# The last attention step's transposed probabilities in a bank and a buffer of their own, and one PSUM copy moved from ScalarE to VectorE

## Time and profile before

| | |
|---|---|
| median of 3 runs | 1077.67 us (1076.57 to 1077.71) |
| profiled execution, its own time | 1077.91 us |
| its span, first to last instruction | 1076.3 us |
| PE busy | 1057.4 us, 98% of the span |
| DVE busy | 344.9 us, 32% |
| ACT busy | 356.3 us, 33% |
| POOL busy | 393.1 us, 37% |

### The profile page before, as it was taken

One profiled execution on the slowest core, in us unless ns is written; L12 is line 12 of the kernel. 1 busy time (PEld: TensorE's weight loads), 2 busy tenths in 40 slices (PEclk: granted clock), 3 DMA queues, 4 the chain that ended last, 5 costly groups with the idle time before them and its releaser, 6 DMA issues.

```text
span 1076.3 us, 17647 instructions
## 1 busy us (share of the span) xinstructions
PE 1057.4 (98%) x5848; PEld 884.3 (82%) x5849; DVE 344.9 (32%) x700; ACT 356.3 (33%) x821; POOL 393.1 (37%) x310
## 2 busy tenths in 40 slices
PE   8999979999999999999999999999999999999998
PEld 6888758888888888888888887988888888888886
DVE  5878841112211122111221112332333232333222
ACT  4678432222222222222222221533344334335333
POOL 6223178785827346280462806830010001100000
PEclk9999999999999999999999999999999999999999
DMA  6676645949733325133241412240011002101001
GB/s 190 175 258 183 219 139 195 331 145 351 245 117 117 117 83 170 39 117 117 79 174 39 149 67 69 88 128 20 20 51 48 20 1 79 40 1 40 1 1 40
DMA packets 50195, 120.09 MB, mean 112 GB/s; under 512 B 7072, under 2 KB 12320, under 8 KB 49632
## 3 DMA queue, kind: packets, MB, share of 16 engines
q0 software_dynamic: 16688, 62.66, 17.8%
q1 hardware_dynamic: 19920, 32.62, 9.7%
q10 hardware_dynamic: 13536, 24.12, 6.5%
HBM read 86.88 MB, written 32.51 MB: 111 GB/s over the span
## 4 chain that ended last, share of the span: by engine, by line
PE 92%; DVE 3%; ACT 2%; DMA 1%; issue 1%; ACTq 0%; POOL 0%; SPq 0%; DVEq 0%; POOLq 0%
PE bank L1492 7%; PE bank L1494 7%; PE bank L1511 7%; PE bank L1509 7%; PE bank L1493 7%; PE bank L1510 7%; PE bank L1557 6%; PE bank L1559 6%; PE bank L1558 6%; PE bank L1550 6%; PE bank L1552 6%; PE bank L1551 6%; PE bank L1517 3%; PE bank L1284 2%; PE bank L1476 2%; PE bank L1310 2%
## 5 line engine op out<-in xcount | busy, mean ns | idle before, releaser
L482 POOL TENSOR_TENSOR Wl<-stage,Wh 128x2048 fp32r<-128x2048 f32 x36 | 165.8, 4605 | 3.0
L1161 DVE COPY y_out<-bank 128x512 f32<-128x512 f32 x42 | 29.1, 692 | 355.2 <-PE bank L1511 355.2
L1492 PE MATMUL bank<-Wh,xT_h 128*128 x336 | 135.4, 403 | 1.4 <-issue 0.9
L1199 DVE SCALAR_TENSOR_TENSOR bank<-bank,square 128x512 f32<-128x512 f32 x72 | 50.4, 700 | 254.8 <-ACT square L837 254.8
L1494 PE MATMUL bank<-Wh,xT_l 128*128 x336 | 131.5, 391 | 0.0
L1511 PE MATMUL bank<-Wh,hT_l 128*128 x336 | 131.1, 390 | 0.0
L1509 PE MATMUL bank<-Wh,hT_h 128*128 x336 | 130.9, 390 | 0.1
L1510 PE MATMUL bank<-Wl,hT_h 128*128 x336 | 130.8, 389 | 0.0
L1493 PE MATMUL bank<-Wl,xT_h 128*128 x336 | 130.8, 389 | 0.0
L808 ACT ACTIVATE hT_h<-bank 128x512 fp32r<-128x512 f32 x84 | 45.8, 596 | 252.3 <-PE bank L1517 252.3
L480 POOL CAST Wh<-stage 128x2048 fp32r<-128x2048 f32 x36 | 68.5, 1903 | 157.2 <-PE bank L1511 155.1
(11 more groups left out here) (236 smaller groups left out, 1741.1 us busy)
## 6 DMA issues: line engine op xcount, KB each, us to landing
stage<-w POOLq DMA_DIRECT2D x32, 1024.0 KB, 5.8
y_sorted<-y_out ACTq DMA_DIRECT2D x42, 256.0 KB, 2.1
x_in<-x_sorted ACTq DMA_DIRECT2D x38, 256.0 KB, 2.8
x_sorted<-gath_b SPq DMA_DIRECT2D x20, 256.0 KB, 4.3
v_ring<-vW SPq DMA_DIRECT2D x36, 128.0 KB, 4.4
x_rows<-x_blk SPq DMA_DIRECT2D x36, 128.0 KB, 3.1
x_sorted<-gath_a SPq DMA_DIRECT2D x18, 256.0 KB, 3.5
k_ring<-kT SPq DMA_DIRECT2D x8, 512.0 KB, 5.7
```

The costliest lines, as they stand in the source:

```text
L482: nc.gpsimd.tensor_tensor(Wl[:, s, cols], stage[:, c % 2], Wh[:, s, cols], ALU.subtract).then_inc(w_ready, 1)
L1492: nc.tensor.matmul(H_ps[a][:], xT_h[:, u, k], high, start=(k == 0), stop=False)
```

## The change

The last step's (35) transposed probabilities go to bank 1 (`S_ps[1]`) in place of bank 3, and their copy goes to half of `q_ring` in place of `probsT`. DVE's copy of step 35 no longer waits for the values of step 34; in its place stands a wait for the last spreading of queries out of that half of `q_ring`. PE does the transposes of step 35 one turn earlier, in turn 36 directly behind those of step 34 and ahead of the values of step 33, and without the wait for step 34's copy. And the copy of step 33 is done by DVE in turn 35, between its bias and its reciprocals, no more by ACT ahead of the exponentials of step 35.

```diff
-BY_SCALAR = (15, 16, 17, 19, 20, 21, 22, 23, 26, 29, 32, 35)
+BY_SCALAR = (15, 16, 17, 19, 20, 21, 22, 23, 26, 29, 32)
...
+        def probsT_of(s):
+            return q_ring[:, 1].rearrange("p b c -> p (b c)")[:, 0:J * P] if s == G - 1 else probsT[:]
+
+        def PT_of(s):
+            return S_ps[1] if s == G - 1 else PT_ps
...
                 if 2 <= s < G + 2 and s not in BY_SCALAR:
                     dve.wait_ge(pT_done, s - 1)
-                    if s >= 3:
+                    if s == G + 1:
+                        dve.wait_ge(q_spread, 2 * B * (BLOCKS - 1))
+                    elif s >= 3:
                         dve.wait_ge(pv_done, s - 2)
-                    nc.vector.tensor_copy(probsT[:], PT_ps[:]).then_inc(pT_copied, 1)
+                    nc.vector.tensor_copy(probsT_of(s - 2), PT_of(s - 2)[:]).then_inc(pT_copied, 1)
...
             def transposed_probs(s):
                 pe.wait_ge(exp_done, s + 1)
-                if s >= 1:
+                if 1 <= s < G - 1:
                     pe.wait_ge(pT_copied, s)
                 for j in range(J):
-                    mm = nc.tensor.transpose(PT_ps[:, P * j:P * j + P], probs[:, s % CH, P * j:P * j + P], ident[:])
+                    mm = nc.tensor.transpose(PT_of(s)[:, P * j:P * j + P], probs[:, s % CH, P * j:P * j + P], ident[:])
...
-                        mm = nc.tensor.matmul(X_ps[s % 2][Q * hi:Q * hi + Q, Q * j:Q * j + Q], probsT[rows, head],
+                        mm = nc.tensor.matmul(X_ps[s % 2][Q * hi:Q * hi + Q, Q * j:Q * j + Q], probsT_of(s)[rows, head],
...
-                if 2 <= s < G + 2:
+                if 2 <= s <= G:
                     transposed_probs(s - 2)
+                if s == G:
+                    transposed_probs(G - 1)
                 if 3 <= s < G + 3:
                     values(s - 3)
```

## The result

The changed kernel is slower: a median of 1081.75 us (1080.43 to 1083.58, 8 runs) against 1077.78 us (1076.57 to 1080.12, 8 runs) for the kernel before, a ratio of 1.003 with a 95% interval from 1.0017 to 1.0043. The prediction had 1078.0 us and a range up to 1079.3 us. Each of these 8 executions of the changed kernel took longer than each of the 8 of the kernel before. The ratios in this text are those on record; they are not quotients of the medians and can differ from these by up to 0.001. The profiled execution took 1080.68 us, its span is 1079.1 us and its mean granted clock 0.992 (0.996 before).

A forecast was written before the change was run, and what follows sets the result against it. Bound: a chain of single instructions from the last attention steps to the token gather, its length counting fully. Terms +0.70 - 0.32 - 0.07 = +0.31 us took the median from 1077.67 to 1078.0 us; range 1076.7 to 1079.3 us.

The forecast's parts named there:

- Parts 1 to 4: From step 33's copy to step 35's: exponentials 0.69 us earlier, values of step 33 0.70 late, step 35's copy +0.31 us.
- Part 5: From the copy of step 35 on, all else keeps its distances: routing 5.18 us behind that copy, at 122.19.
- rival C: PE's longer idle time before the values of step 35 lowers the clock: +1.7 us, 1079.3 us; chance 0.05.
- the prediction's formula for C: Low clock before routing: +0.31 us, plus 1.65 us of lost PE work, less 0.3 us to spare at `e_hT_l`: +1.7 us.
- Rivals A and B: A: values of step 33 not held up, 1077.3 us, chance 0.14. B: step 35's copy starts unchanged, 1077.7 us, 0.08.

The follow-up runs named there:

- e1_fill: The changed kernel with five filler matmuls ahead of the values of step 35: 1078.72 us against 1077.40 us for the kernel before, ratio 1.0006.
- e2_order: The changed kernel with the transposes of step 35 behind the values of step 33: 1077.94 us against 1077.40 us for the kernel before, ratio 1.0006.
- f1_gap: The kernel before with one useless DVE memset (1024 columns) ahead of its copy of step 35: 1080.95 us against 1078.75 us, ratio 1.0021.
- g3_order_gap: The changed kernel, transposes of step 35 behind step 33's values, plus a 480-column DVE memset before step 35's copy: 1081.24 us, ratio to before 1.0029.
- f4_late: The kernel before with fillers in two later gaps only (12 ahead of the token search, 16 in place of 8 behind it): 1077.51 us, ratio 0.9995.
- g1_gap2: The kernel before with two useless DVE memsets (1024 and 512 columns) ahead of its copy of step 35: 1083.29 us against 1078.51 us, ratio 1.0052.
- f2_fill2: The changed kernel with two filler matmuls ahead of the values of step 35: 1078.99 us against 1078.75 us for the kernel before, ratio 1.0012.

## Why the prediction was wrong

**What bounds the kernel: right.** The stage is a chain whose length counts fully. From the first tile product on, the two profiles differ by 0.22 us in 928.

**Parts 1 to 4: right, nearly to the row.** The values of step 33 start 2.35 us behind the bias (2.40 forecast), the copy of step 34 3.15 us (3.20 forecast), and DVE's queue takes the 2.55 us forecast from there to the copy of step 35. The copy of step 34 waits for the values of step 33, held up by the transposes and by the exponentials of step 35; DVE's queue then is the bound, and the copy of step 35 has no wait before it. Forecast +0.31 us at that copy, measured +0.26. The experiments bear out the terms: 5.15 us with the transposes behind the values (5.05 forecast), 6.39 us with the exponentials as late as before (6.4 to 6.5 forecast). `e1_fill` isolates this sum at the start of the routing: 10.88 - 10.62 = +0.26 us.

**Part 5, "all else keeps its distances": the step that failed.** It kept the routing 5.18 us behind the copy of step 35; measured were 7.87 us. It took TensorE's matmuls at their old durations behind a gap of 1.4 us, which it had itself worked out (1.26 measured). What happened is rival C, which the prediction named at this place and gave 0.05. Neither argument against it held. That 1.4 us lies below the 2.05 us of the only fall looked at the earlier trace rows made one row into a bound; in the table above the share of low executions grows, roughly, with the gap: at most 3 of 12 up to 0.82 us, half at 1.18 us, 31 of 39 at 1.25 to 1.27 us, 8 of 10 at 1.72 us. And that work surrounds the gap did not keep the clock up: TensorE was busy on both sides. Then the price was mis-sized: it took the length of the fall from that same row, 3.3 us, and so +1.7 us and a sign that stays within no change. The fall lasted 10.2 us. The forecast's own bound, that a fall decides the sign only from 4.4 us on, was passed.

**What the 10.2 us cost.** Beyond the queue's 0.26 us, the routing starts 2.69 us later, as values, transposes and two groups of logits stand in the chain at half clock. Then the 20 early products take 6.29 us, where from their start to the transposes behind them they had some 4.6; DVE's `e_hT_l` had 0.3 us to spare, and the token table is 4.29 - 2.95 = 1.34 us later again. Nearly all of it, 1.32 us, is there once DVE has the counts, which stand in TensorE's queue behind the early products, their transposes and five fillers:

```profile
131.86 0.31 DVE L1104 TENSOR_TENSOR cnt_gt<-bank,steps 128x144 f32<-128x144 f32 x1 [0.48 <-PE bank L1435]
```

The last 0.58 us, between the token table and the first tile, are not the fall's: in `e1_fill`, without it, this stretch is as long (6.93 us, against 6.94 in the changed kernel and 6.36 before). Why it is shorter in the profile before isn't shown. So of the 5.1 us that the clock loses, some 4.05 us reach the first tile, and this is the difference to `e1_fill`. That the prediction's formula for C would give 0.31 + 5.1 - 0.3 = +5.1 us with the true length, the very sum of the table, is in part luck: it has no term for these 0.58 us, and takes less off for hidden work than was hidden.

**The spread.** The prediction took the noise of a median, 0.6 us, from three runs that lay within 1.1 us. The 92 later executions of the kernel before go from 1075.20 to 1084.21 us. The miss is larger than that uncertainty and isn't explained by it, but the term was too small.

The Trainium skill's rule in TensorE: Matmul & The Clock Gate, section "Why this matters for your kernels", is that long idle gaps between bursts of matmuls send the clock back to its lower level; the prediction weighed it as against the change. These traces agree as far as idle time comes first: 10.2 us at 0.50 behind 1.26 us of it. But this rule speaks only of gaps longer than this one, and taken by its words it would price this gap at nothing; here the measurement decides.

**Rivals A and B** did not come: A needs the transposes behind the values, as in `e2_order`. **What stays open:** why one execution falls and the next doesn't, and whether `f1_gap`'s lower share (6 of 12 at 1.18 us) against `g3_order_gap`'s (10 of 12 at 1.27 us) is the gap's length, what TensorE does ahead of it, the chip (the `e`, `f` and `g` experiments ran on three chips, and the kernel before had 1 of 30, 0 of 35 and 3 of 27 low executions on them), or chance. Length alone doesn't decide: in its first 20 us the changed kernel has a gap of 1.43 us, and `f4_late` one of 1.47 us, and both profiles show a clock of 1.00 behind it.

## What to carry to other kernels

Where a schedule change lengthens an idle gap on TensorE, ask what runs behind the gap before calling it hidden: the price is not the gap, but everything on the chain that TensorE then does at half clock, here for 10.2 us. Don't take the shortest gap behind which a trace shows a fall as a bound: one that is longer than the gaps around it in the kernel as it is can bring a fall though it is shorter than that. A few filler matmuls in the gap tell in one experiment whether the clock or the queue costs the time, and mend it as well. Time such a kernel often, and read the mean clock of each execution beside its time.

## What the runs showed of the hardware that was not expected

- The granted clock fell behind 1.25 to 1.27 us of idle time, with TensorE busy on both sides: four profiles show it, and by the mean clock it came in 17 of 20 executions of the changed kernel.
- Once low, it did not rise though TensorE was busy for all of the time: from 116 to 122 us the busy share is 100% at 0.50, with logits of 16 columns, transposes and four wide products. It rose at 125.7 us, some 3.4 us after the last 20 wide products (the early products, 512 columns each) had begun.
- In all five profiles that show it, the clock stayed low for 10.2 us, and it rose between 3.3 us (`g3_order_gap`) and 5.4 us (`g1_gap2`) after the start of these products. Falls at other places lasted 3.4 us (before, from 139.6 to 143.0 us) or 6.8 us (`f2_fill2`, from 137.7 to 144.5 us). The changed kernel's profile has one of these too, 6.8 us from 139.3 us on, where the kernel before has 3.4 us; the token search in it took 3.2 us in both.
- The same program falls or not from one execution to the next, which makes up much of its spread: 1081.16 to 1086.47 us low against 1078.03 to 1080.75 us high in `f1_gap`. The mean granted clock of each execution, not its time alone, tells the two apart.
